# First five pairs of a linear-attention lead-in: order of tail copies, row squares, key exponentials and one quotient

## The chip, the core and the metric

The kernel runs on one core of a Trainium2 chip. The core's engines work side by side and wait for each other through semaphores: TensorE (PE in the rows; PEld is its weight load), VectorE (DVE), ScalarE (ACT), GpSimd (POOL) and SyncE (SP, which here only issues transfers). The metric is the device time of one execution in microseconds (us), lower is better.

## The reference

Random-feature attention over 4 batches x 8 heads, 576 tokens, head size 64, 128 features, followed by two feed-forward layers over all 2304 tokens of width 512 and inner width 2048:

```python
def phi(x):
    proj = np.einsum('bhsd,md->bhsm', x, omega)
    sq = np.sum(x * x, axis=-1, keepdims=True) / 2.0
    h = proj - sq
    h = h - np.max(h, axis=-1, keepdims=True)
    return np.exp(h) / np.sqrt(m)
q_p, k_p = (phi(q_s), phi(k_s))
kv = np.einsum('bhsm,bhsd->bhmd', k_p, v)
z = np.sum(k_p, axis=2)
num = np.einsum('bhsm,bhmd->bhsd', q_p, kv)
den = np.einsum('bhsm,bhm->bhs', q_p, z)[..., None] + 1e-06
...
x = x @ w_in;  g = x * clip(x + 3, 0, 6) / 6;      x = g @ w_out     # first layer
x = x @ w_in2; g = x / (1 + exp(-1.702 * x));      x = g @ w_out2    # second layer
```

## The kernel before

Two heads that lie together are a pair; there are 16. A pair has 576 tokens: four tiles of 128 for each head and a tail of 64, whose two heads share one tile. The feed-forward layers take the tokens in five chunks (four of 512, one of 256) and the inner width in 16 blocks; block `n` has `hidden(n)` (x by w_in) and `output(n)` (g by w_out), each product written as three matmuls of rounded halves (`x_hi`, `x_lo`, `w_hi`, `w_lo`). The four pairs of a batch make up the width of 512, so the first chunk (the first 512 tokens of batch 0) needs pairs 0 to 3 whole. They run in a lead-in with most of pair 4 (`LEAD = 5`), and the rest of pair 4 and pairs 5 to 15 are spread over slots between the blocks.

Each engine runs its own list, written out by hand in one function per engine; what is written is what is issued, and an instruction waits at its place for its semaphores while everything behind it on that engine waits too. For a pair `a` in the lead-in the steps are:

- PE `projection(a, u)` for u = "q", "k" and "tail" (L482, L475): q into banks acc0 and acc1, k into acc2 and acc3, tail into hid0. The next pair's projection waits until the exponentials have read the bank.
- DVE `statistics(a, u)`: row maxima (L864, L861), then two small instructions, `h_max` (L879) and `bias` (L882). Both read two small tiles in SBUF. The half norms they read come from squared rows: ACT squares them (`square_rows`, L671), and for pairs 2 to 4 GpSimd folds them (`fold_rows`, L397 and L399) after both kinds of the pair are squared.
- ACT `exps` (L690, four tiles for each head; L684, the tail), then PE `turn(a, h)` (L504) transposes the query features of head `h`, and ACT `turned_head(a, h)` (L696) copies them back to SBUF.
- PE `key_values(a)` (L510 to L519): transposes the query tail, and for a > 0 the 64 tail tokens of the result of pair a-1 (L513), then sums keys by values. DVE `keep(a)` (L897, L899) copies the sums and the turned tail; `take_tails(a-1)` (L937) copies the pair a-1 tails into `X`.
- PE `quotient(a)` (L533, L536) makes numerators and denominators, DVE `quotient(a)` (L913 to L928) divides, PE `turn_back(a)` (L543) transposes the result, ACT `first_high(a)` (L701) and DVE `first_low(a)` (L942) split it into `x_hi` and `x_lo`.

On PE, `turn(a+1, 0)` waits for `tails_out` and for `take_tails(a-1)`, since it writes over the bank in which the old tails lie. Pair 3 is followed by pieces of `hidden(0, ...)`, which run between `quotient(3)`, the two turns of pair 4, `turn_back(3)` and pair 4's tail projection. `output(0)` writes acc0 to acc3, so it waits bank by bank for pair 4's exponentials: the third and fourth banks hold its key projection. From there on ACT's list per block is `gate(n)` (L753), `high(n)` (L762), attention pieces, and `high_weights` (L729), and DVE's is `gated_block(n)` (L973), attention pieces and `low(n)` (L980).

## Time and profile before

| | us |
|---|---|
| median of three runs | 948.0 |
| lowest and highest of them | 945.12 and 948.49 |
| the profiled execution | 947.79 |
| span between its first and last instruction | 944.9 |
| PE busy within the span | 935.7 |

The span is what the views cover; 2.9 us of the profiled execution lie outside it. Times in a view count from the span's start. In a timeline row the first number is the start, the second the length, and the bracket holds the idle time ahead of it on that engine with what ended it. A matmul's end is modelled, so rows of PE overlap a little and the pitch from one start to the next is the better measure. PEclk is the granted TensorE clock, 1.00 for 2.4 GHz and 0.50 for 1.2 GHz.

### The profile page before, as it was taken

How to read it: one execution, taken by the hardware profiler on the slowest of the kernel's cores; microseconds unless marked ns; L12 is line 12 of the kernel's file. 1: busy time of each engine (PE TensorE's matmuls, PEld its weight loads, DVE VectorE, ACT ScalarE, POOL GpSimd, SP SyncE). 2: the span in 40 equal slices, each digit the busy share in tenths (PEclk: the TensorE clock that was granted, in tenths of full speed). 3: DMA queues.
4: the chain of work that ended last, by engine and by line, in shares of the span. 5: the costliest groups of instructions: out<-in, count | busy, mean ns of one | idle time of the engine just before them, and what ended most of it. 6: DMA issues, size and time to landing. Idle time of an engine off the chain costs nothing.

```text
span 944.9 us, 12973 instructions
## 1 busy us (share of the span) xinstructions
PE 935.7 (99%) x5126; PEld 784.7 (83%) x5126; DVE 398.1 (42%) x734; ACT 381.1 (40%) x871; POOL 170.2 (18%) x182
## 2 busy tenths in 40 slices
PE   8999999999999999999999999999999999999998
PEld 7878788887888778888889988888888888888898
DVE  6856654655546554452224442232223222422332
ACT  7665654554445544442225742232223222322322
POOL 2647455221221210000005830000000000000000
PEclk9999999999999999999999999999999999999999
DMA  8534432212121111010003510001001000100010
GB/s 268 151 89 150 126 106 63 62 39 63 26 63 51 51 26 38 1 45 1 1 0 93 178 43 1 1 1 45 0 1 45 1 1 0 45 1 1 7 39 24
DMA packets 40731, 45.99 MB, mean 49 GB/s; under 512 B 21600, under 2 KB 22240, under 8 KB 40672
## 3 DMA queue, kind: packets, MB, share of 16 engines
q1 hardware_dynamic: 40304, 44.54, 15.5%
q8 instruction: 41, 0.67, 0.3%
q10 hardware_dynamic: 368, 0.62, 0.2%
q14 instruction: 18, 0.15, 0.0%
HBM read 40.44 MB, written 4.72 MB: 48 GB/s over the span
## 4 chain that ended last, share of the span: by engine, by line
PE 97%; DVE 2%; ACT 1%; issue 0%; DVEq 0%
PE acc L616 14%; PE acc L618 14%; PE acc L617 14%; PE hid L593 11%; PE hid L597 10%; PE hid L594 10%; PE att L597 4%; PE att L593 4%; PE att L594 4%; PE att L519 3%; PE att L482 3%; PE att L561 2%; PE att L504 2%; PE acc L482 1%; PE att L475 1%; DVE row_max L864 1%
## 5 line engine op out<-in xcount | busy, mean ns | idle before, releaser
L616 PE MATMUL acc<-g_hi,w_out_hi 128*128 128x512 f32 (+1 forms) x640 | 241.5, 377 | 0.1
L618 PE MATMUL acc<-g_hi,w_out_lo 128*128 128x512 f32 (+1 forms) x640 | 236.2, 369 | 0.0
L617 PE MATMUL acc<-g_lo,w_out_hi 128*128 128x512 f32 (+1 forms) x640 | 235.9, 369 | 0.0
L593 PE MATMUL hid<-x_hi,w_in_hi 128*128 128x512 f32 (+1 forms) x476 | 181.6, 381 | 0.0
L597 PE MATMUL hid<-x_lo,w_in_hi 128*128 128x512 f32 (+1 forms) x476 | 176.0, 370 | 0.4 <-DVE x_lo L965 0.4
L594 PE MATMUL hid<-x_hi,w_in_lo 128*128 128x512 f32 (+1 forms) x476 | 175.4, 369 | 0.0
L980 DVE TENSOR_TENSOR g_lo<-R,g_hi 128x512 fp32r<-128x512 f32 (+1 forms) x160 | 109.0, 681 | 92.4 <-ACT g_hi L762 92.4
L616 PEld LDWEIGHTS acc<-g_hi,w_out_hi 128*128 128x128 f32 x640 | 120.8, 189 | 21.8 <-issue 2.4
L618 PEld LDWEIGHTS acc<-g_hi,w_out_lo 128*128 128x128 f32 x640 | 120.6, 188 | 20.4
L617 PEld LDWEIGHTS acc<-g_lo,w_out_hi 128*128 128x128 f32 x640 | 120.8, 189 | 19.6
L762 ACT ACTIVATE g_hi<-R 128x512 fp32r<-128x512 f32 (+1 forms) x160 | 94.6, 591 | 84.3 <-DVE R L975 52.5
L973 DVE SCALAR_TENSOR_TENSOR R<-R,hid 128x512 f32<-128x512 f32 (+1 forms) x79 | 49.9, 631 | 130.1 <-ACT R L753 130.1
L593 PEld LDWEIGHTS hid<-x_hi,w_in_hi 128*128 128x128 f32 x476 | 89.8, 189 | 16.9 <-issue 0.2
L597 PEld LDWEIGHTS hid<-x_lo,w_in_hi 128*128 128x128 f32 x476 | 89.7, 188 | 16.3 <-DVE x_lo L965 0.8
L594 PEld LDWEIGHTS hid<-x_hi,w_in_lo 128*128 128x128 f32 x476 | 89.8, 189 | 14.4
L753 ACT ACTIVATE R<-hid 128x512 f32<-128x512 f32 (+1 forms) x79 | 43.9, 556 | 106.4 <-PE hid L597 106.3
L975 DVE TENSOR_TENSOR R<-R,hid 128x512 f32<-128x512 f32 (+1 forms) x40 | 25.4, 634 | 113.5 <-ACT R L755 113.5
L975 DVE TENSOR_TENSOR R<-R,att 128x512 f32<-128x512 f32 (+1 forms) x40 | 25.4, 634 | 113.0 <-ACT R L755 113.0
L755 ACT ACTIVATE R<-att 128x512 f32<-128x512 f32 (+1 forms) x40 | 22.2, 555 | 117.0 <-PE att L597 116.4
L755 ACT ACTIVATE R<-hid 128x512 f32<-128x512 f32 (+1 forms) x40 | 22.2, 555 | 116.4 <-PE hid L597 116.4
L948 DVE RECIPROCAL k_phi<-k_phi 128x288 f32<-128x288 f32 x24 | 46.8, 1949 | 38.4 <-ACT k_phi L708 38.4
L594 PE MATMUL att<-x_hi,w_in_lo 128*128 128x512 f32 (+1 forms) x164 | 60.4, 368 | 0.0
(144 smaller groups left out, 1047.9 us busy)
## 6 DMA issues: line engine op xcount, KB each, us to landing
X<-w_in SPq DMA_DIRECT2D x16, 256.0 KB, 2.7
X<-w_out SPq DMA_DIRECT2D x16, 256.0 KB, 2.9
out_t<-X SPq DMA_DIRECT2D x16, 256.0 KB, 2.2
q_cols<-q_t SPq DMA_DIRECT2D x14, 288.0 KB, 2.9
k_cols<-k_t SPq DMA_DIRECT2D x14, 288.0 KB, 3.6
rows<-q_n SPq DMA_DIRECT2D x13, 288.0 KB, 3.6
rows<-k_n SPq DMA_DIRECT2D x13, 288.0 KB, 3.2
v_rows<-v_n SPq DMA_DIRECT2D x14, 256.0 KB, 3.3
```

What stands on the lines that cost most here:

```text
L593: nc.tensor.matmul(bank, w_hi[0][:, at], x_hi[:, k, x0:x0 + t], start=(k == 0), stop=False)
L594: nc.tensor.matmul(bank, w_lo[0][:, at], x_hi[:, k, x0:x0 + t], start=False, stop=False)
L597: last = nc.tensor.matmul(bank, w_hi[0][:, at], x_lo[:, k, x0:x0 + t], start=False, stop=(k == KC - 1))
L616: nc.tensor.matmul(bank, w_hi[1][:, at], g_hi[:, g, 0:t], start=(s == 0), stop=False)
L617: nc.tensor.matmul(bank, w_hi[1][:, at], g_lo[:, g, 0:t], start=False, stop=False)
L618: last = nc.tensor.matmul(bank, w_lo[1][:, at], g_hi[:, g, 0:t], start=False, stop=(s == J - 1))
L755: nc.scalar.activation(R[:, 0:t], h, ACT.Sigmoid, scale=1.702).then_inc(gate_ready, 1)
L762: nc.scalar.activation(g_hi[:, n % G_SLOTS, 0:t], R[:, 0:t], ACT.Copy).then_inc(g_hi_ready, 1)
L948: nc.vector.reciprocal(d, d).then_inc(recip_done, 1)
L973: nc.vector.scalar_tensor_tensor(out=r, in0=r, scalar=6.0, in1=h, op0=ALU.min, op1=ALU.mult).then_inc(gated, 1)
L975: nc.vector.tensor_tensor(r, r, h, ALU.mult).then_inc(gated, 1)
L980: nc.vector.tensor_tensor(g_lo[:, n % G_SLOTS, 0:t], R[:, 0:t], g_hi[:, n % G_SLOTS, 0:t].bitcast(F32), ALU.subtract).then_inc(g_ready, 1)
```

## The change

Five things are moved or recut, all of them in the lead-in; the arithmetic stays.

- DVE copies the old tails (`take_tails`) right behind `keep`, ahead of the key statistics. Pair 4's key statistics move behind `first_low(3)`. For pair 1 the query statistics come ahead of the key maxima.
- ACT squares one kind of rows ahead of `first_high(a)` and the other behind it, both ahead of the next query exponentials. In the start the tail exponentials of pair 0 come ahead of its turned heads.
- ACT takes the key exponentials of a pair in one piece, with the turned heads and the tail behind them; pair 4's come behind `high(0)`. On PE the next key projection moves ahead of `turn(a+1, 1)`.
- PE runs `turn_back(3)` ahead of `turn(4, 1)`, and ACT runs `first_high(3)` ahead of that head's copy.
- DVE's quotient handles the tails first; for pair 3 it is done head by head, with a reciprocal for each.

```diff
--- before.py
+++ after.py
@@ -638,16 +638,16 @@
                 quotient(a)
                 turn(a + 1, 0)
                 projection(a + 2, "q")
+                projection(a + 2, "k")
                 turn(a + 1, 1)
-                projection(a + 2, "k")
                 turn_back(a)
             key_values(LEAD - 2)
             hidden(0, (0,))
             quotient(LEAD - 2)
             turn(LEAD - 1, 0)
             hidden(0, (1,))
+            turn_back(LEAD - 2)
             turn(LEAD - 1, 1)
-            turn_back(LEAD - 2)
             projection(LEAD - 1, "tail")
             hidden(0, (2, 3))
             for n in range(2 * L2):
@@ -785,29 +785,28 @@
             square_rows(0, KK)
             exps_of(0, "q")
             exps_of(0, "k")
+            exps_of(0, "tail")
+            square_rows(1, KQ)
             turned_head(0, 0)
             turned_head(0, 1)
-            exps_of(0, "tail")
-            for a in (1, 2):
-                square_rows(a, KQ)
-                square_rows(a, KK)
+            square_rows(1, KK)
+            square_rows(2, KQ)
+            square_rows(2, KK)
             exps_of(1, "q")
             for a in range(LEAD - 2):
-                exps(a + 1, "k", 0)
+                exps_of(a + 1, "k")
                 turned_head(a + 1, 0)
-                exps(a + 1, "k", 1)
+                exps_of(a + 1, "tail")
                 turned_head(a + 1, 1)
-                exps_of(a + 1, "tail")
-                first_high(a)
-                exps_of(a + 2, "q")
                 if a + 3 < LEAD:
                     square_rows(a + 3, KQ)
+                first_high(a)
+                if a + 3 < LEAD:
                     square_rows(a + 3, KK)
-            exps(LEAD - 1, "k", 0)
+                exps_of(a + 2, "q")
             turned_head(LEAD - 1, 0)
+            first_high(LEAD - 2)
             turned_head(LEAD - 1, 1)
-            first_high(LEAD - 2)
-            exps(LEAD - 1, "k", 1)
             for n in range(2 * L2):
                 former, now = slot_units(2 * n - 1), slot_units(2 * n)
                 for a, what in former:
@@ -833,6 +832,7 @@
                 if n == L2 - 1:
                     nc.scalar.activation(spare[:], ident[:, 0:1], ACT.Sigmoid)
                 if n == 0:
+                    exps_of(LEAD - 1, "k")
                     exps_of(LEAD - 1, "tail")
                 for a, what in now:
                     if what not in ("nd0", "nd1"):
@@ -908,25 +908,34 @@
                 return slice(h * D, (h + 1) * D), slice(at, at + D), slice(at + D, at + D + 1)
 
             def quotient(a):
+
                 tiles = [num_bank(a, h)[:, 0:ST * (D + 1)].rearrange("p (t c) -> p t c", t=ST) for h in range(2)]
-                dve.wait_ge(nd_done, 4 * a + 2)
-                nc.vector.tensor_scalar(dens[:, 0:ST], tiles[0][:, :, D], EPS, None, ALU.add)
-                for h in range(2):
-                    rows_h, _, den = tail_of(h)
-                    nc.vector.tensor_scalar(dens[rows_h, 2 * ST:GROUPS], num_bank(a, 0)[rows_h, den], EPS, None, ALU.add)
-                dve.wait_ge(nd_done, 4 * a + 4)
-                nc.vector.tensor_scalar(dens[:, ST:2 * ST], tiles[1][:, :, D], EPS, None, ALU.add).then_inc(dens_set, 1)
-                dve.wait_ge(dens_set, a + 1)
-                nc.vector.reciprocal(dens[:], dens[:]).then_inc(dens_ready, 1)
-                dve.wait_ge(dens_ready, a + 1)
-                if a > 0:
-                    dve.wait_ge(xs_turned, a)
-                for h in range(2):
-                    rows_h, num, _ = tail_of(h)
-                    nc.vector.tensor_tensor(xs[:, 0:ST, h * D:(h + 1) * D], tiles[h][:, :, 0:D],
-                                            dens[:, h * ST:(h + 1) * ST].unsqueeze(2).to_broadcast([P, ST, D]), ALU.mult)
-                    last = nc.vector.tensor_tensor(xs[rows_h, ST, h * D:(h + 1) * D], num_bank(a, 0)[rows_h, num],
-                                                   dens[rows_h, 2 * ST:GROUPS].to_broadcast([D, D]), ALU.mult)
+                dens_at = (slice(0, ST), slice(ST + 1, GROUPS))
+                tails = slice(ST, ST + 1)
+                parts = ((0,), (1,)) if a == LEAD - 2 else ((0, 1),)
+                for i, heads in enumerate(parts):
+                    for h in heads:
+                        dve.wait_ge(nd_done, 4 * a + 2 * h + 2)
+                        if h == 0:
+                            for side in range(2):
+                                rows_h, _, den = tail_of(side)
+                                nc.vector.tensor_scalar(dens[rows_h, tails], num_bank(a, 0)[rows_h, den], EPS, None, ALU.add)
+                        last = nc.vector.tensor_scalar(dens[:, dens_at[h]], tiles[h][:, :, D], EPS, None, ALU.add)
+                    last.then_inc(dens_set, 1)
+                    dve.wait_ge(dens_set, a + i + 1)
+                    d = dens[:, 0 if 0 in heads else ST + 1:ST + 1 if 1 not in heads else GROUPS]
+                    nc.vector.reciprocal(d, d).then_inc(dens_ready, 1)
+                    dve.wait_ge(dens_ready, a + i + 1)
+                    if a > 0 and i == 0:
+                        dve.wait_ge(xs_turned, a)
+                    for h in heads:
+                        if h == 0:
+                            for side in range(2):
+                                rows_h, num, _ = tail_of(side)
+                                nc.vector.tensor_tensor(xs[rows_h, ST, side * D:(side + 1) * D], num_bank(a, 0)[rows_h, num],
+                                                        dens[rows_h, tails].to_broadcast([D, D]), ALU.mult)
+                        last = nc.vector.tensor_tensor(xs[:, 0:ST, h * D:(h + 1) * D], tiles[h][:, :, 0:D],
+                                                       dens[:, dens_at[h]].unsqueeze(2).to_broadcast([P, ST, D]), ALU.mult)
                 last.then_inc(xs_ready, 1)
 
             def take_tails(a):
@@ -1004,26 +1013,26 @@
                 biases(0, u)
             statistics(0, "tail")
             maxima(1, "q")
-            maxima(1, "k")
             norms(1, KQ)
             biases(1, "q")
+            maxima(1, "k")
             keep(0)
             norms(1, KK)
             biases(1, "k")
             for a in range(LEAD - 2):
                 if a > 0:
                     keep(a)
+                    take_tails(a - 1)
                     statistics(a + 1, "k")
-                    take_tails(a - 1)
                 statistics(a + 1, "tail")
                 quotient(a)
                 statistics(a + 2, "q")
                 first_low(a)
             keep(LEAD - 2)
             take_tails(LEAD - 3)
-            statistics(LEAD - 1, "k")
             quotient(LEAD - 2)
             first_low(LEAD - 2)
+            statistics(LEAD - 1, "k")
             for n in range(2 * L2):
                 before, former, now = (slot_units(2 * n - i) for i in (2, 1, 0))
                 for a, what in former:
```

VectorE, from the copy of pair 1's sums (`keep(1)`) through the key statistics of pair 2 to its tail statistics; L937 and L946 are the copy of the old tails:

```order
 L897 COPY state<-att 128x130
 L899 COPY q_tail_phi_b<-att 128x128
-L864 TENSOR_REDUCE row_max<-acc 128x4 x2
-L879 SCALAR_TENSOR_TENSOR h_max<-row_max,half_norm 128x8
-L882 SCALAR_TENSOR_TENSOR bias<-h_max,half_norm 128x8
-L937 COPY X<-att 64x64 x2
+L946 COPY X<-att 64x64 x2
+L864 TENSOR_REDUCE row_max<-acc 128x4 x2
+L879 SCALAR_TENSOR_TENSOR h_max<-row_max,half_norm 128x8
+L882 SCALAR_TENSOR_TENSOR bias<-h_max,half_norm 128x8
 L861 TENSOR_REDUCE row_max<-hid 128x2
```

The tail copy now stands ahead of three statistics steps instead of behind them; the same happens one pair later.

ScalarE, from the copy of the turned head of pair 1 to the first steps of pair 2 (L671 with X is the squaring of pair 3's rows):

```order
-L690 ACTIVATE k_phi_b<-acc,bias 128x128 x4
-L696 ACTIVATE q_phi_b<-att 128x512
-L690 ACTIVATE k_phi_b<-acc,bias 128x128 x4
+L690 ACTIVATE k_phi_b<-acc,bias 128x128 x8
 L696 ACTIVATE q_phi_b<-att 128x512
 L684 ACTIVATE q_tail_phi_b<-hid,bias 128x128
 L684 ACTIVATE k_phi_b<-hid,bias 128x128
+L696 ACTIVATE q_phi_b<-att 128x512
+L671 ACTIVATE X<-X 128x576
 L701 ACTIVATE x_hi<-att 128x512
+L671 ACTIVATE X<-X 128x576
 L690 ACTIVATE q_phi<-acc,bias 128x128 x8
```

The eight key exponentials stand together, and the two squarings stand on both sides of `x_hi`'s copy instead of behind the query exponentials.

TensorE, in the cycle that turns pair 2 and projects pair 3 (L482 with X):

```order
 L504 MATMUL att<-ident,q_phi 128x128 x4
-L482 MATMUL acc<-omega,X 128x128 x8
+L482 MATMUL acc<-omega,X 128x128 x16
 L504 MATMUL att<-ident,q_phi 128x128 x4
-L482 MATMUL acc<-omega,X 128x128 x8
 L543 MATMUL att<-ident,x_by_token 128x128 x4
 L510 MATMUL att<-ident,q_tail_phi 128x128
```

Both projections now stand between the two turns.

## Rows read from the trace of the kernel before

**Rows 1.** The page's first part: busy time, share of the span, instructions of each engine.

```profile
PE 935.7 (99%) x5126; PEld 784.7 (83%) x5126; DVE 398.1 (42%) x734; ACT 381.1 (40%) x871; POOL 170.2 (18%) x182
```

**Rows 2.** Busy time of the engines by stretch, with granted clock and transfers.

```profile
core 0: us, PE busy (x) PEld busy (x) DVE busy (x) ACT busy (x) POOL busy (x), PEclk, DMA share, GB/s
...
29.60:33.00 3.40, 3.29 (x22) 2.77 (x23) 2.79 (x13) 2.38 (x8) 3.01 (x7) 0.50 0.58 180
...
58.20:944.90 886.70, 883.36 (x4669) 739.29 (x4669) 356.09 (x607) 340.75 (x754) 148.04 (x146) 1.00 0.13 39
```

**Rows 3.** Waits of PE: what for, us in total, times, longest.

```profile
PE att L504 <- ACT q_phi L696: 0.6, 1, 0.6
...
PE att L510 <- ACT k_phi L684: 0.2, 1, 0.2
```

**Rows 4.** Timeline of PE, from the end of quotient(1) to key_values(2).

```profile
27.64 1.00 PE L533 MATMUL att<-state,q_phi_b 128*128 128x65 f32 x8
29.71 1.09 PE L504 MATMUL att<-ident,q_phi 128*128 128x128 f32 x4 [1.07 <-DVE X L937]
30.73 2.08 PE L482 MATMUL acc<-omega,X 64*128 64x128 f32 x16
32.74 0.75 PE L504 MATMUL att<-ident,q_phi 128*128 128x128 f32 x4
...
35.00 0.27 PE L510 MATMUL att<-ident,q_tail_phi 128*128 128x128 f32 x1
```

**Rows 5.** Timeline of PE, the same cycle one pair later.

```profile
39.16 1.00 PE L533 MATMUL att<-state,q_phi 128*128 128x65 f32 x8
41.23 0.63 PE L504 MATMUL att<-ident,q_phi_b 128*128 128x128 f32 x4 [1.07 <-DVE X L937]
41.79 1.16 PE L482 MATMUL acc<-omega,q_cols 64*128 64x128 f32 x16
42.89 0.66 PE L504 MATMUL att<-ident,q_phi_b 128*128 128x128 f32 x4
...
45.26 0.27 PE L510 MATMUL att<-ident,q_tail_phi_b 128*128 128x128 f32 x1
```

**Rows 6.** Timeline of DVE behind key_values(1).

```profile
25.86 0.29 DVE L897 COPY state<-att 128x130 f32<-128x130 f32 x1 [0.86 <-PE att L519]
...
27.65 1.33 DVE L879 SCALAR_TENSOR_TENSOR h_max<-row_max,half_norm 128x8 f32<-128x8 f32 x1
29.01 0.17 DVE L882 SCALAR_TENSOR_TENSOR bias<-h_max,half_norm 128x8 f32<-128x8 f32 x1
29.09 0.47 DVE L937 COPY X<-att 64x64 f32<-64x64 f32 x2
29.59 0.42 DVE L861 TENSOR_REDUCE row_max<-hid 128x2 f32<-128x256 f32 x1
```

**Rows 7.** Timeline of ACT: eight key exponentials, row squares, half the next pair's key exponentials.

```profile
10.82 2.17 ACT L690 ACTIVATE k_phi<-acc,bias 128x128 f32<-128x128 f32 x8
...
26.17 1.31 ACT L671 ACTIVATE X<-X 128x576 f32<-128x576 f32 x2
29.21 1.14 ACT L690 ACTIVATE k_phi<-acc,bias 128x128 f32<-128x128 f32 x4 [1.73 <-DVE bias L882]
```

**Rows 8.** Timeline of POOL, the first step of folding pair 3's rows.

```profile
27.56 1.39 POOL L397 TENSOR_TENSOR X<-X 128x576 f32<-128x576 f32 x1 [2.98 <-ACT X L671]
```

**Rows 9.** Timeline of PE: the second turn of pair 4, and key_values(4).

```profile
52.11 0.63 PE L504 MATMUL att<-ident,q_phi 128*128 128x128 f32 x4 [0.55 <-ACT q_phi L696]
...
61.05 0.27 PE L510 MATMUL att<-ident,q_tail_phi 128*128 128x128 f32 x1
```

**Rows 10.** Timeline of DVE: the low half of pair 3's result, and the gate of block 0.

```profile
53.90 0.69 DVE L942 TENSOR_TENSOR x_lo<-att,x_hi 128x512 fp32r<-128x512 f32 x1 [1.70 <-ACT x_hi L701]
56.02 0.69 DVE L973 SCALAR_TENSOR_TENSOR R<-R,hid 128x512 f32<-128x512 f32 x1 [1.43 <-ACT R L753]
```

**Rows 11.** Timeline of ACT: the high half of block 0, and the gate of block 1.

```profile
56.74 0.63 ACT L762 ACTIVATE g_hi<-R 128x512 fp32r<-128x512 f32 x1 [0.75 <-DVE R L973]
...
59.10 0.59 ACT L753 ACTIVATE R<-att 128x512 f32<-128x512 f32 x1
```

## The prediction

> **What bounds the kernel now.** I read the page's first part, then the busy time by stretch, then PE's own timeline where it is not full. PE is busy 99% of the span [rows 1], and from 58.20 on it is idle 3.3 us in 886.7 [rows 2]. Nothing in that long part is touched but the place of a few ScalarE steps in the first blocks, so the change can be worth only what PE loses in the 58 us ahead of it. That is little: 944.9 - 935.7 = 9.2 us are idle in all, and 3.3 of these lie behind the lead-in, so 5.9 us are idle within it, some 1 us of that before the first instruction. Added to this is one stretch in which PE is busy but slow: from 29.6 to 33.0 the granted clock is 0.50, that is 1.2 GHz, with 1.00 before and behind [rows 2].
>
> The largest waits of PE in the lead-in are the first turn of pair 2 and that of pair 3: each stands 1.07 us until VectorE's copy of the old tails is made (L937) [rows 4, 5]. VectorE makes that copy as the last of four things [rows 6]: the sums at 25.86, the key maxima, h_max and bias until 29.18, and only then the copy at 29.09 to 29.56. These rows are the place at which the change has its effect; the 0.55 us ahead of pair 4's second turn [rows 9] and the 0.2 us ahead of the first key_values [rows 3] are the small ones.
>
> **Part 1: the first pair.** ScalarE's tail exponentials of pair 0 come ahead of its turned heads, so the 0.2 us for which PE's L510 waits go [rows 3]. ScalarE has the same work up to the query exponentials of pair 1, only permuted; VectorE gets the query statistics of pair 1 ready while it would wait. PE's work in the next cycle is the same, and its new wait for all key exponentials of pair 1 is about what the old gap between turn and projection was. Value: -0.25, between 0 and -0.5.
>
> **Part 2: pair 2's turn.** Before, from the end of quotient(1) at 27.64 + 1.00 = 28.64 to key_values(2) at 35.00 are 6.36 us [rows 4]. It holds the wait of 1.07 and the slow clock. The same steps one pair later take 41.23 to 45.26 = 4.03 us at 2.4 GHz, a gap of 0.13 among them [rows 5], so the work itself is 3.9. The price of the slow clock is what the pitches differ by: 29.71 to 30.73 is 1.02 against 0.56, 30.73 to 32.74 is 2.01 against 1.10, and the last turn 0.75 against 0.66 [rows 4, 5]: 0.46 + 0.91 + 0.09 = 1.46 us.
>
> After the change the copy stands behind the sums. From keep's start at 25.86, keep takes 0.4 and the copy 0.5, so it is made at 26.8, while PE is in quotient(1) until 28.64: the wait of 1.07 is gone. What is late next is the key projection of pair 3, which now stands ahead of the second turn and needs all eight key exponentials of pair 2. The chain, in the clock of before: maxima from 26.8 on; from 26.27 they took until 27.65 (the start of h_max, 25.86 + 0.4 is their start), 1.38, so h_max starts at 28.15. h_max and bias take 0.2 each when nothing holds them, the second as in its row [rows 6], so bias is ready at 28.5. ScalarE has been free since the query exponentials and starts within 0.05; eight exponentials take 2.17 [rows 7], until 30.7, and PE follows 0.15 later, at 30.9. PE itself has turned pair 2 and projected its query columns by 28.64 + 0.56 + 1.10 = 30.3, plus a first gap of 0.05. The new wait is therefore 0.5 us. Behind it come the second turn and turn_back, for which the turned head's copy (0.5) and VectorE's quotient are in time.
>
> h_max is not free of risk. Before it took 1.33 us from 27.65 to 28.98 instead of 0.2 [rows 6], and GpSimd's first fold step of pair 3 ran from 27.56 to 28.95 [rows 8]: the two end together. Bias and row maxima next to it kept their length, so I read this as VectorE's instruction with two small inputs in SBUF being held until GpSimd's step ends. The Trainium skill says in "GPSIMD Engine Reference", section 1, Specifications, that GpSimd shares its SBUF interfaces with VectorE and contends with VectorE instructions that have two SBUF inputs. The trace agrees, and adds the size: 1.33 us for one.
>
> This is where the squares matter. The fold starts when ScalarE has squared both kinds. Before, that was behind the query exponentials: 26.17 + 1.31 = 27.5 [rows 7], and the long fold step fell right on h_max. Now the squares lie around x_hi's copy, ahead of the query exponentials that took 2.1 us; the fold starts near 25.3, its step of 1.39 [rows 8] ends near 26.8, before h_max at 28.15, and only the shorter steps behind it can meet h_max and bias. That is 0 to 0.5 us more wait; I take 0.2, so the new wait is 0.7. The query exponentials of pair 2 end 1.3 us later, but PE's turn needs the first half of them only by 28.7 and has it by 26.5.
>
> Cycle after: 3.9 + 0.7 = 4.6 against 6.36: **-1.75**. Of this 1.46 hang on the clock: I count the stretch at 1.2 GHz as gone, since PE had stood still for 1.07 us right ahead of it, and now nothing stands still there. The same idle of 1.07 one pair later did not bring the clock down [rows 5], so idle time alone does not decide, and this is the least safe part of the sum.
>
> **Part 3: pair 3's turn.** Before, from 39.16 + 1.00 = 40.16 to 45.26 are 5.10 us [rows 5], at full clock. After, the same chain gives 4.6: **-0.5**. If h_max and bias meet no fold step it is -0.7, if they meet two it is -0.2.
>
> **Part 4: pair 3's quotient and pair 4.** The wait of 0.55 ahead of pair 4's second turn came from ScalarE, which had the first half of the key exponentials (1.14) ahead of the turned head. Now turn_back(3) stands first and waits for VectorE's quotient. VectorE no longer has pair 4's key statistics (some 1.8 us) ahead of it, but it cannot start before PE has made the numerators; by head it starts 0.8 us earlier and pays one more reciprocal with its handshake (0.25), and its end comes out near 52.0 where it was 52.2. PE stands there 0.6 us, as before: **0**, between -0.3 and +0.3. Behind it, pair 4's key statistics must fit between x_lo and the gate of block 0: x_lo from about 53.4 (53.90 before) for 0.7, then 1.8 us, end near 55.9, against a gate at 56.02 [rows 10]. It fits with 0.1 to spare; what is over comes onto output(0) one to one, 0 to +0.4.
>
> ScalarE now has pair 4's key exponentials behind g_hi: 56.74 + 0.55 + 2.17 = 59.5, and the tail by 60.1. output(0) writes the third accumulator 1.5 us and the fourth 2.2 us behind its start at 58.2, and needs the two halves at 58.4 and 59.5, so it is covered by over 0.8; key_values(4) at 61.05 [rows 9] is covered by 0.9. The gate of block 1 goes from 59.10 [rows 11] to about 61.2, two weight halves with it, and through VectorE's gate to numerators(4) and output(1), which PE reaches at 66 and 68: covered by over 1 us. I cost it at nothing.
>
> **Sum.** -0.25 - 1.75 - 0.5 + 0 = -2.5 us. Against the profiled execution, 947.79 (944.9 of span and 2.9 around it), that is **945.3 us**. The profiled execution is 0.2 under the median of 948.0, so I use it as it is. One of the three runs, 945.12, already lies 2.9 under the median; that spread is as large as the whole effect, and a run without the slow stretch would explain 1.46 of it.
>
> **Rivals.** (a) The slow clock stays or comes elsewhere. For it speaks that the idle ahead of it explains it only once in two cases; the new wait of 0.7 could do the same. Then 1.46 come back: 946.8. (b) The waits only change their name. If the key exponentials end later than I work out, by 0.9 per pair, from x_hi's and VectorE's order together, the two new waits are 1.6 each; with the clock gone this gives 945.3 + 1.8 = 947.1, with it 948.6. (c) Slower: VectorE's h_max and bias are both held by long GpSimd steps. With the fold elsewhere, GpSimd's weight halves follow, of about the length of the long fold step. Two holds of 1.3 make the new wait 0.5 + 2.6 = 3.1 in each of the two cycles instead of 0.7, so 945.3 + 4.8 = 950.1. It decides from a mean wait of 0.7 + 2.5 / 2 = 1.95 per cycle on, above which the kernel is slower than before. Against it: both would need to fall on a long step twice, and the long fold step is moved away. (d) The change does more: no hold at all, and the start's slow phase happens to end earlier, as in the run of 945.12. This gives under 943.5. (e) It does not do what it says: PE's turn waits for something else in place of the copy, such as the query exponentials, which are 1.3 later than before. They are ready 2 us ahead of the turn, so this has hardly a chance of its own and goes with (b).
>
> **How the numbers follow.** The forecast, 944.2 to 946.2, has 0.55; (a) 0.22; (b) with (e) 0.12; (c) 0.06; (d) 0.05. The range of 943.5 to 947.6 holds the forecast, (a) and half of (b), and leaves out (c), most of (d) and the rest of (b), under 2 in 10. A measurement of this kernel can tell about 0.5% from no change, 4.7 us. PE's idle time in the lead-in and the slow stretch together are 7 us, and less than 4 of them are touched, so faster by over 0.5% (under 943.3) has 0.05; slower by over 0.5% (over 952.7) needs (c) and slow stretches besides, 0.02; the rest is within, 0.93.
>
> **What would show it.** Right: no wait of L504 for the tail copy, in its place one of the key projection (L482) for the key exponentials of 0.5 to 1.0 us, twice; the fold of pair 3 about 2 us earlier and h_max near 0.2 to 0.5 us; PEclk 1.00 from 26 to 45; key_values(3) at about 42.8 instead of 45.26; the gate of block 0 about 2.5 us earlier than 56.02, straight behind pair 4's key statistics. Wrong: a stretch at 0.50, an h_max over 1 us with the fold or a weight half beside it, PE waiting at key_values(4) or in output(0), or a PE idle time after the first block other than 3.3 us.

## The result

The changed kernel takes 943.8 us (median of 12 runs, 943.67 to 944.36), the kernel before 945.89 (12 runs, 944.77 to 948.91). The ratio is 0.997, with an interval from 0.9959 to 0.9981: faster by 0.3%, which the interval sets apart from no change, but less than the 0.5% that I had called the least that can be told. The time is 1.5 us under the forecast of 945.3: it lies in the outer range of 943.5 to 947.6, but below the 944.2 to 946.2 in which I expected it. Repeated beside three experiments the changed kernel took 944.43 (12 runs, 943.72 to 944.89; ratio 0.9978, 0.997 to 0.9987).

A second thing changed, and it is needed to read the numbers. The runs of the kernel before lie in two groups: five of these 12 between 948.0 and 948.9, seven between 944.8 and 946.0, nothing between. In the last comparison it was 7 of 23 above 947.8. The changed kernel has one group, 24 runs of 24 below 944.9 (counting the repetition). The execution that I predicted from, 947.79, is of the upper group.

The busy time by stretch of the changed kernel (columns as in [rows 2]) shows that the stretch at 1.2 GHz is gone. The profiled execution took 943.76, its span is 941.3.

```profile
26.00:29.60 3.60, 3.31 (x36) 2.95 (x35) 3.21 (x14) 2.49 (x11) 3.13 (x8) 1.00 1.02 283
29.60:33.00 3.40, 2.90 (x33) 2.81 (x33) 2.85 (x7) 2.48 (x8) 2.70 (x3) 1.00 0.58 189
...
55.00:941.30 886.30, 882.90 (x4669) 738.85 (x4667) 354.97 (x607) 342.30 (x760) 147.28 (x146) 1.00 0.13 39
```

PE's idle time behind the lead-in is 3.4 us, where it was 3.3 [rows 2]: all of the difference lies ahead of it. Its waits, changed kernel (what for, us in total, times, longest):

```profile
PE acc L482 <- ACT k_phi L690: 1.3, 2, 0.8
...
PE acc L482 <- ACT k_phi_b L690: 1.0, 2, 0.8
PE att L543 <- DVE x_by_token L937: 0.5, 1, 0.5
```

The waits for the tail copy are gone. In their place stands one of 0.8 in each cycle for the key exponentials, at the key projection (the rest of these two rows, 0.5 and 0.2, is ahead of the two cycles), and 0.5 for the divided tokens where there were 0.55 for the turned head [rows 9]. PE's timeline of the cycle of [rows 4], and the two key_values behind it:

```profile
26.77 1.00 PE L533 MATMUL att<-state,q_phi_b 128*128 128x65 f32 x8
27.61 0.61 PE L504 MATMUL att<-ident,q_phi 128*128 128x128 f32 x4
28.15 1.16 PE L482 MATMUL acc<-omega,X 64*128 64x128 f32 x16
30.10 1.16 PE L482 MATMUL acc<-omega,X 64*128 64x128 f32 x16 [0.79 <-ACT k_phi L690]
31.20 0.65 PE L504 MATMUL att<-ident,q_phi 128*128 128x128 f32 x4
31.69 0.60 PE L543 MATMUL att<-ident,x_by_token 128*128 128x128 f32 x4
32.12 0.27 PE L510 MATMUL att<-ident,q_tail_phi 128*128 128x128 f32 x1
...
41.64 0.27 PE L510 MATMUL att<-ident,q_tail_phi_b 128*128 128x128 f32 x1
```

The turn follows the quotient without a gap. Behind the key_values of pair 3, at 41.64, PE reaches output(0) after 12.93 us (12.95 before), and from there both kernels take 886.7 us.

### The profile page after: what moved, and what is told of

Read it like the earlier page. It is cut to its first block, busy times and chain, and to the rows that moved or that the text cites. A ratio compares the mean times of both kernels' runs of the same rounds, so it can differ in the third digit from the quotient of the medians.

```text
span 941.3 us, 12974 instructions
## 1 busy us (share of the span) xinstructions
PE 932.8 (99%) x5126; PEld 782.8 (83%) x5126; DVE 394.3 (42%) x735; ACT 380.5 (40%) x871; POOL 169.9 (18%) x182
## 4 chain that ended last, share of the span: by engine, by line
PE 96%; DVE 2%; ACT 2%; issue 0%; DVEq 0%
PE acc L616 14%; PE acc L617 14%; PE acc L618 14%; PE hid L593 11%; PE hid L597 10%; PE hid L594 10%; PE att L593 4%; PE att L594 4%; PE att L597 4%; PE att L519 3%; PE att L482 3%; PE att L561 2%; PE att L504 1%; PE att L475 1%; DVE row_max L864 1%; PE acc L482 0%
## 5 line engine op out<-in xcount | busy, mean ns | idle before, releaser
L616 PE MATMUL acc<-g_hi,w_out_hi 128*128 128x512 f32 (+1 forms) x640 | 241.5, 377 | 0.1
L616 PEld LDWEIGHTS acc<-g_hi,w_out_hi 128*128 128x128 f32 x640 | 120.7, 189 | 21.8 <-issue 2.4
L593 PE MATMUL att<-x_hi,w_in_hi 128*128 128x512 f32 (+1 forms) x164 | 60.4, 368 | 0.0
```

The lines of the kernel that those rows point to most:

```text
L593: nc.tensor.matmul(bank, w_hi[0][:, at], x_hi[:, k, x0:x0 + t], start=(k == 0), stop=False)
L616: nc.tensor.matmul(bank, w_hi[1][:, at], g_hi[:, g, 0:t], start=(s == 0), stop=False)
```

## A ruler for the experiments

The first key_values starts at a time that varies by up to 1 us from one execution of a kernel order to the next, and by 2.2 us in the profiled execution of tails_alone; the first transfers and the speed of the first projection (16 matmuls in 1.29 us in b_again, in 1.99 in tails_alone) differ already. So each profiled execution is also read from key_values(0) to the start of output(0), with the cycles between key_values(1), (2) and (3), all as starts of L510 and of the first L616 in PE's timeline:

| kernel | median, us | cycle 1 to 2 | cycle 2 to 3 | key_values(0) to output(0) |
|---|---|---|---|---|
| before, upper group ([rows 3 to 5, 9]) | 948.2 | 11.52 | 10.26 | 43.68 |
| before, lower group (b_again) | 945.7 | 10.26 | 9.17 | 41.62 |
| changed | 943.8 | 9.51 | 9.52 | 40.80 |
| tails_alone | 946.50 | 10.14 | 10.14 | 42.18 |
| squares_old | 945.40 | 10.13 | 10.14 | 42.03 |
| split_exps | 944.18 | 9.47 | 9.47 | 40.81 |
| fourth_old | 944.36 | 9.50 | 9.52 | 40.78 |
| tails_old | 942.95 | 8.93 | 8.95 | 39.66 |
| maxima_tails_old | 942.94 | 8.45 | 9.12 | 39.35 |
| maxima_early | 942.43 | 8.45 | 8.45 | 38.67 |
| maxima_all | 942.12 | 8.45 | 8.45 | 38.24 |

(For the two groups of before, the times are the medians of the 28 and 58 runs of each group that were taken beside the experiments. The other medians come from different chips, so differences of a few tenths are read from the last column.) One unit of the last column is one unit of time: what lies behind output(0) is 886.7 to 886.8 us in all.

Two things stand outside this ruler. From the first turn to key_values(0) the kernel before takes 4.7 us (9.84 to 14.53, and 9.86 to 14.56 in b_again), the changed kernel 4.4 (9.38 to 13.77): another 0.3 of gain, which is part 1's. And the time outside the span is 2.35 to 2.63 us in all 24 runs of the changed kernel, but 2.73 to 3.03 in 77 of 86 runs of the kernel before, and in 6 of 8 runs of fourth_old below. No run shows where these 0.4 us come from.

## Experiments on the kernel before

**b_again**: the kernel before, once more and without an edit, to catch an execution of the other group.

> The kernel before, unchanged. Its twelve runs so far lie in two groups, five between 948.0 and 948.9 and seven between 944.8 and 946.0; the changed kernel's twelve lie between 943.7 and 944.4. Theory: the upper group is the executions with a stretch at 1.2 GHz behind the 1.07 us wait of the first turn (the profiled one of before had it from 29.6 to 33.0). Then the two groups appear again, and a profiled execution of about 945.4 shows no such stretch, while one of about 948.4 does. Rival: the groups come from elsewhere (start, transfers); then both kinds of profile look alike in PEclk.

12 runs, median 945.83 (945.39 to 948.48), two of them above 947.4. The mean granted clock of every run, kept with its time, ties the groups to the clock: of the 86 runs of the kernel before that were taken here and beside the other experiments, the 28 with a mean of 0.998 are exactly those from 947.58 up, and the 58 with 0.999 or 1.000 lie at 946.58 or below. The profiled one took 945.83. PE in the cycle of [rows 5], which there had 1.07 of waiting for the tail copy:

```profile
37.93 1.00 PE L533 MATMUL att<-state,q_phi 128*128 128x65 f32 x8
38.84 0.63 PE L504 MATMUL att<-ident,q_phi_b 128*128 128x128 f32 x4
39.40 1.16 PE L482 MATMUL acc<-omega,q_cols 64*128 64x128 f32 x16
```

DVE and POOL beside it, with the query bias that comes earlier on DVE:

```profile
34.15 1.15 DVE L882 SCALAR_TENSOR_TENSOR bias<-h_max,half_norm 128x8 f32<-128x8 f32 x1
...
37.93 0.17 DVE L879 SCALAR_TENSOR_TENSOR h_max<-row_max,half_norm 128x8 f32<-128x8 f32 x1
38.14 0.17 DVE L882 SCALAR_TENSOR_TENSOR bias<-h_max,half_norm 128x8 f32<-128x8 f32 x1
38.22 0.47 DVE L937 COPY X<-att 64x64 f32<-64x64 f32 x2
```

```profile
34.00 1.27 POOL L417 TENSOR_TENSOR w_out_lo<-X,w_out_hi 128x512 fp32r<-128x512 f32 x1
38.73 3.59 POOL L397 TENSOR_TENSOR rows<-rows 128x576 f32<-128x576 f32 x5 [3.45 <-ACT rows L671]
```

The clock is 1.00 throughout this execution. The first cycle has its wait of 1.07 as before and is 1.26 shorter than in the upper group; that is the price of the slow stretch (I had 1.46). But the second cycle is 1.09 shorter as well, and nothing in it is slow: h_max takes 0.17 because the fold begins 0.8 behind it, and so the copy is made in time. Counted from key_values(2), h_max starts at 4.17 in the execution of [rows 5] and at 4.16 here, but the fold at 4.08 there (39.08) and at 4.96 here. The fold follows ScalarE's query exponentials, and here these waited for a query bias that one of GpSimd's weight halves held until 35.30. GpSimd keeps its pace while PE is slow (the weight half at 32.06 in the one and at 32.10 in the other take 1.26 us each): in the execution of [rows 5] the one that holds the bias here started 1.04 us ahead of key_values(2) (33.96), here 0.23 behind it, and so it met another instruction. So a stretch at 1.2 GHz in the first cycle costs its own 1.26 and then 1.09 for a wait that it brings about in the next, of which 0.29 comes back behind key_values(3) (12.95 us to output(0) against 13.24 here): 2.06 in all. The same 1.07 stood in both cycles of my rows, and I took it for a property of the kernel.

**fill_wait** and **fill_short**: the kernel before with matmuls on PE in the wait ahead of the turn.

```diff
                 quotient(a)
+                if a > 0:                 # fill_short: if a == 1
+                    pe.wait_ge(exp_done, banks_to(a + 1, "q", 1))
+                    warm(8, acc[0])       # fill_short: warm(4, acc[0])
                 turn(a + 1, 0)
```

> The kernel before with eight idle-filling matmuls of 128 columns (about 0.13 us each) on PE ahead of the first turn of pair 2 and of pair 3, where it waits 1.07 us; they write a bank that is free then, and no order is changed. Theory (idle PE ahead of the turn brings the clock down): the waits cost the same, but the upper group is gone, all runs 945.0 to 946.2, PEclk 1.00 from 26 to 45. Rival (the stretch has another cause): two groups as in the kernel before, some runs over 948.

12 runs, median 947.63 (946.96 to 950.07), ratio 1.002 (1.001 to 1.0029). Neither expectation fits. Eight fillers take 1.84 us (28.10 to 29.94), not 1.07, and the second cycle had no wait to hide them in: both cycles are 10.83 or 10.84. The times alone don't tell whether a group is missing; the granted clock does in part: eleven of the twelve have a mean of 1.000 and one, 950.07, has 0.998, where 28 of 86 would have been about four. The filler has to fit.

> The kernel before with four filling matmuls of 128 columns on PE ahead of pair 2's first turn only, where it waits 1.07 us in both kinds of execution (29.71 and 29.74). Eight of them took 1.84 us from first start to the turn, so four take about 0.92 and fit into the wait. Theory (the idle there brings the clock to 1.2 GHz in part of the executions, and the upper group is these): no run, or one of twelve, above 947.4, where the kernel before has some 4 in 10, and a median of 945.4 to 946.0. Rival (the upper group has another cause): 4 or 5 of twelve above 947.4.

12 runs, median 946.16, 945.45 to 947.28, none above 947.4, where the kernel before had 7 of 23 beside it on the same chip. PE's timeline:

```profile
28.17 1.11 PE L491 MATMUL acc<-state 128*128 128x128 f32 x8
29.40 0.63 PE L504 MATMUL att<-ident,q_phi 128*128 128x128 f32 x4
```

The turn starts when it did, and its stretch from key_values(0) to output(0) is 41.62, as in b_again. What is taken away is only the idle time, and with it the upper group. All twelve have a granted clock of 1.000. With 28 of 86 runs in the upper group, twelve without one would come up by chance about once in a hundred times (an estimate from these two counts). That is the evidence that PE's idle time ahead of this turn brings on the slow stretch, in a part of the executions. What tells these from the others was not found; the upper end of this kernel's runs, 947.28, lies higher than the lower group's.

**tails_alone**: of the whole change only the tail copy is moved.

```diff
                     keep(a)
+                    take_tails(a - 1)
                     statistics(a + 1, "k")
-                    take_tails(a - 1)
```

> The kernel before with one part of the change alone: the old tails are copied right behind the sums. Theory of the prediction's sum (the copy is what PE waits for): the two waits of 1.07 go, about 2 us less than the lower group of before, 943.4. Rival (the chain of key statistics and key exponentials stands right behind it and takes the wait over; the copy alone also delays that chain by 0.5, while the fold's long step still lies on h_max): at most 0.3 us per cycle is gained, 944.9 to 945.5, with PE waiting for exponentials at the key projection instead. Either way the upper group should be gone if the idle ahead of the turn makes the clock drop, since the idle moves behind a projection.

12 runs, median 946.5 (945.87 to 948.56), ratio 0.9996 (0.9987 to 1.0006). The rival was right that the copy's move gains nothing, but its 944.9 to 945.5 was too low. Both cycles are 10.14, their sum 20.28 against 19.43 in b_again; 0.29 of these 0.85 comes back behind key_values(3), and to output(0) 0.56 is lost. Eleven of the twelve runs have a granted clock of 1.000. The twelfth, 948.56, is the profiled one: its slow stretch lies not here but at the start, behind 1.99 us in which PE waited for the first key columns (6.57 to 8.56), and the ruler does not hold it.

```profile
9.00:14.00 5.00, 5.00 (x40) 4.38 (x38) 2.95 (x8) 4.36 (x17) 0.00 (x0) 0.66 1.02 288
```

PE's waits:

```profile
PE att L504 <- ACT q_phi L696: 1.4, 2, 0.8
...
PE att L504 <- ACT q_phi_b L696: 0.8, 1, 0.8
...
PE acc L482 <- ACT k_phi L690: 0.4, 1, 0.4
PE acc L482 <- ACT k_phi_b L690: 0.4, 1, 0.4
```

VectorE's h_max in the first cycle:

```profile
30.38 0.84 DVE L879 SCALAR_TENSOR_TENSOR h_max<-row_max,half_norm 128x8 f32<-128x8 f32 x1
```

In the first cycle the copy ahead of the statistics costs nothing: h_max starts 0.5 later than in b_again but is held to the end of the same fold step, and counted from key_values(1) (25.71 here, 23.51 there) the key exponentials start at 5.75 (31.46) against 5.74 (29.25). PE's wait only changes its name, and the cycle is 0.12 shorter. In the second cycle the half microsecond moves h_max from ahead of the fold (b_again) to under it (0.83 in place of 0.17), and the cycle is 0.97 longer.

## Experiments on the changed kernel

**changed_again**: the changed kernel without an edit; its result is given above.

> The changed kernel, unchanged, beside the three others on one chip. 943.8 with one group of runs, 943.6 to 944.6; both theories of the other runs take it as their base.

**tails_old**: the tail copy back behind the key statistics, all else as changed.

```diff
                     keep(a)
-                    take_tails(a - 1)
                     statistics(a + 1, "k")
+                    take_tails(a - 1)
```

> The changed kernel with the tail copy put back behind the key statistics, all else as changed. Theory of the sum (the copy bound the turn): PE waits about 1 us for the copy again at both turns, 945.8. Rival (with the squares moved, h_max is short, so the copy would be made only 0.3 us after PE arrives, and the key exponentials start 0.5 us earlier than in the changed kernel): PE waits 0.35 at the turn and hardly at the key projection, 943.8 - 0.9 = 942.9 to 943.4.

5 runs, median 942.95 (942.77 to 943.54), ratio to the kernel before 0.996 (0.9948 to 0.9973). The rival by its number, though PE's wait at the turn is 0.1 where it had 0.35. VectorE:

```profile
25.45 1.28 DVE L864 TENSOR_REDUCE row_max<-acc 128x4 f32<-128x512 f32 x2
26.84 0.19 DVE L879 SCALAR_TENSOR_TENSOR h_max<-row_max,half_norm 128x8 f32<-128x8 f32 x1
27.06 0.17 DVE L882 SCALAR_TENSOR_TENSOR bias<-h_max,half_norm 128x8 f32<-128x8 f32 x1
27.14 0.47 DVE L946 COPY X<-att 64x64 f32<-64x64 f32 x2
```

The copy is made at 27.61 and PE's turn starts at 27.75, 0.1 later than the changed kernel's relative to key_values(1). From the start of the first projection to the second turn PE then takes 28.31 to 30.68 = 2.37, where the changed kernel takes 28.15 to 31.20 = 3.05. Each cycle is 0.57 to 0.58 shorter. So the part of the change that I had put in its centre costs 1.1 us here, where h_max is short: as tails_alone shows, it costs nothing while h_max is held to the same step's end.

**squares_old**: both squarings back behind the query exponentials.

```diff
-                if a + 3 < LEAD:
-                    square_rows(a + 3, KQ)
                 first_high(a)
+                exps_of(a + 2, "q")
                 if a + 3 < LEAD:
+                    square_rows(a + 3, KQ)
                     square_rows(a + 3, KK)
-                exps_of(a + 2, "q")
```

> The changed kernel with both squarings back behind the next query exponentials. Theory (a fold step of 1.39 us that falls on h_max holds it): the fold starts near 26.8 and h_max at 27.3 ends with its first step near 28.2; the two waits for exponentials grow from 0.79 to about 1.5, 943.8 + 1.4 = 945.2, x_hi's copy being earlier without use. Rival (the hold is chance or harmless): 943.8 within 0.3.

11 runs, median 945.4 (945.08 to 946.12), ratio 0.9984 (0.9975 to 0.9993). By the number of the theory. DVE and POOL:

```profile
28.30 0.88 DVE L878 SCALAR_TENSOR_TENSOR h_max<-row_max,half_norm 128x8 f32<-128x8 f32 x1
29.21 0.17 DVE L881 SCALAR_TENSOR_TENSOR bias<-h_max,half_norm 128x8 f32<-128x8 f32 x1
```

```profile
27.75 1.40 POOL L397 TENSOR_TENSOR X<-X 128x576 f32<-128x576 f32 x1 [2.62 <-ACT X L671]
```

h_max ends at 29.18, the fold's step at 29.15, and PE waits 1.41 for the exponentials in each cycle. The place of the squares is worth 1.23 us from key_values(0) to output(0), about as much as the changed kernel gains over the lower group.

**split_exps**: key exponentials in two halves around the turned head, PE's second turn ahead of the key projection.

```diff
-                exps_of(a + 1, "k")
+                exps(a + 1, "k", 0)
                 turned_head(a + 1, 0)
-                exps_of(a + 1, "tail")
+                exps(a + 1, "k", 1)
                 turned_head(a + 1, 1)
+                exps_of(a + 1, "tail")
...
-                projection(a + 2, "k")
                 turn(a + 1, 1)
+                projection(a + 2, "k")
```

> The changed kernel with the key exponentials of pairs 1 to 3 again in two halves around the turned head, and PE's second turn again ahead of the key projection. Theory: the end of the chain is the same, since the copy of the turned head (0.5 us) only changes place with a turn on PE (0.5 us): 943.6 to 944.1. Rival (one piece matters): 0.5 us per cycle slower, 944.8.

9 runs, median 944.18 (943.87 to 945.13), ratio 0.9979 (0.9969 to 0.9988). No difference beyond that of the runs: PE waits 0.16 and 0.40 in place of 0.79, and the cycles are 9.47.

**fourth_old**: quotient(3) in one piece and everything of pair 4 in its old order, on PE, ScalarE and VectorE.

```diff
             hidden(0, (1,))
-            turn_back(LEAD - 2)
             turn(LEAD - 1, 1)
+            turn_back(LEAD - 2)
...
+            exps(LEAD - 1, "k", 0)
             turned_head(LEAD - 1, 0)
-            first_high(LEAD - 2)
             turned_head(LEAD - 1, 1)
+            first_high(LEAD - 2)
+            exps(LEAD - 1, "k", 1)
...
                 if n == 0:
-                    exps_of(LEAD - 1, "k")
...
-                parts = ((0,), (1,)) if a == LEAD - 2 else ((0, 1),)
+                parts = ((0, 1),)
...
+            statistics(LEAD - 1, "k")
             quotient(LEAD - 2)
             first_low(LEAD - 2)
-            statistics(LEAD - 1, "k")
```

> The changed kernel with everything of pairs 3 and 4 behind keep(3) as before: quotient in one piece, key statistics of pair 4 ahead of it, second turn ahead of turn_back, key exponentials of pair 4 ahead of the gate of block 0. Theory (one wait of 0.5 us for another): 943.8 within 0.2. Rival (the part gains on its own): 944.2 to 944.5.

8 runs, median 944.36 (943.95 to 945.09), ratio 0.9977 (0.9966 to 0.9987). No difference that can be measured: 40.78 to output(0) against 40.80, with the old wait of 0.6 for the turned head in place of 0.5 for the tokens.

## A faster version

The new wait ends a chain of maxima, h_max, bias and eight exponentials, while VectorE stands idle for 1.07 us ahead of first_low. **maxima_early** puts the maxima there, for pairs 2 and 3:

```diff
                     take_tails(a - 1)
-                    statistics(a + 1, "k")
+                    biases(a + 1, "k")
...
                 statistics(a + 2, "q")
+                if a < LEAD - 3:
+                    maxima(a + 2, "k")
                 first_low(a)
```

> The changed kernel with one more move: VectorE takes the row maxima of the next pair's keys ahead of first_low, in an idle of 1 us there, for pairs 2 and 3; h_max and bias stay behind the tail copy. Theory (the new waits of 0.79 at the key projection are the end of the chain maxima, h_max, bias, eight exponentials): the chain is 1.3 us shorter, the two waits go, 943.8 - 1.5 = 942.3, perhaps 0.1 to 0.3 of it lost since x_lo comes a little later. Rival (the wait is set by ScalarE's query exponentials that end at 26.5, or h_max then falls on the fold's long step at 24.7 to 26.1): half of it or less, 943.0 to 943.8.

6 runs, median 942.43 (941.48 to 942.66), ratio to the kernel before 0.9954 (0.9941 to 0.9967). Both cycles are 8.45, and PE waits in neither:

```profile
27.91 0.61 PE L504 MATMUL att<-ident,q_phi 128*128 128x128 f32 x4
28.44 2.06 PE L482 MATMUL acc<-omega,X 64*128 64x128 f32 x32
30.43 0.65 PE L504 MATMUL att<-ident,q_phi 128*128 128x128 f32 x4
```

**maxima_all** does the same for pair 4, in VectorE's idle ahead of first_low(3), and lets PE's second turn go ahead of turn_back(3) again, since it is ready first.

```diff
             hidden(0, (1,))
-            turn_back(LEAD - 2)
             turn(LEAD - 1, 1)
+            turn_back(LEAD - 2)
...
-            first_high(LEAD - 2)
             turned_head(LEAD - 1, 1)
+            first_high(LEAD - 2)
...
             quotient(LEAD - 2)
+            maxima(LEAD - 1, "k")
             first_low(LEAD - 2)
-            statistics(LEAD - 1, "k")
+            biases(LEAD - 1, "k")
```

> The kernel maxima_early with two more moves around pair 4: the second turn again ahead of turn_back(3) on PE, with its copy ahead of first_high(3) on ScalarE, and the row maxima of pair 4's keys ahead of first_low(3) on VectorE, in its idle of 1.4 us. Theory (PE stands 0.5 us for the divided tokens while the turn could run, and the gate of block 0 must not be delayed by the key statistics): 0.4 us under maxima_early, 942.0. Rival (the end of the chain through x_hi, x_lo is what counts): the same as maxima_early, 942.4.

5 runs, median 942.12 (941.32 to 942.37), ratio 0.9951 (0.9936 to 0.9966), against 944.43 for the changed kernel on the same chip. From key_values(0) to output(0) it is 38.24, 0.43 under maxima_early, as expected; the medians of five and six runs differ by 0.3, which they can't carry alone. VectorE around the moved maxima:

```profile
47.14 1.28 DVE L864 TENSOR_REDUCE row_max<-acc 128x4 f32<-128x512 f32 x2
48.63 0.69 DVE L951 TENSOR_TENSOR x_lo<-att,x_hi 128x512 fp32r<-128x512 f32 x1 [0.21 <-ACT x_hi L701]
```

**maxima_tails_old** is maxima_early with the tail copy behind h_max and bias.

```diff
-                    take_tails(a - 1)
                     biases(a + 1, "k")
+                    take_tails(a - 1)
```

> The kernel maxima_early with the tail copy behind h_max and bias instead of ahead of them. Theory (which of the two stands first matters only while one of them is what PE waits for; with the maxima early PE waits for neither): the same as maxima_early, 942.4 within 0.3. Rival (the tail copy belongs behind the key statistics in any case, as the gain of tails_old over the changed kernel suggests): 0.3 or more lower.

5 runs, median 942.94 (942.36 to 943.43), ratio 0.9961 (0.9946 to 0.9976). Both expectations miss. The first cycle is 8.45, the second 9.12, with a wait that no other kernel has:

```profile
35.42 1.08 PE L533 MATMUL att<-state,q_phi 128*128 128x65 f32 x8 [0.72 <-DVE q_tail_phi L899]
```

VectorE and POOL ahead of it:

```profile
31.96 1.17 DVE L882 SCALAR_TENSOR_TENSOR bias<-h_max,half_norm 128x8 f32<-128x8 f32 x1
33.05 1.28 DVE L864 TENSOR_REDUCE row_max<-acc 128x4 f32<-128x512 f32 x2
34.25 0.68 DVE L951 TENSOR_TENSOR x_lo<-att,x_hi 128x512 fp32r<-128x512 f32 x1
34.85 0.28 DVE L897 COPY state<-att 128x130 f32<-128x130 f32 x1
```

```profile
31.83 1.27 POOL L417 TENSOR_TENSOR w_out_lo<-X,w_out_hi 128x512 fp32r<-128x512 f32 x1
```

The query bias of pair 3 is held until a weight half ends (33.13 and 33.10). The maxima, x_lo and the copy of the sums stand behind it, and now that the maxima fill VectorE's idle time there is none left to take it up. In maxima_early the same bias started before that weight half, at 31.40, and took 0.17. The traces show what put it there: counted from key_values(1), the fold's first step starts at 2.07 in both kernels, but h_max at 3.28 in maxima_early, behind the tail copy, and at 2.78 here. It is held to the end of that step in both, for 0.22 there and 0.71 here, and VectorE reaches the tail statistics of pair 2 at 3.74 there and at 4.11 here. So the tail copy ahead of h_max is of use in this kernel: it is done in time that h_max would spend held. At pair 3's query bias 0.14 us of that delay is left (0.18 behind key_values(2) against 0.04), just enough to come behind the start of the weight half and into the next hold, which shows that the faster versions have little room there.

## Why the prediction came out as it did

Against the profiled execution that it was made from, point by point (starts in PE's timeline):

| step | forecast | measured |
|---|---|---|
| first pair, up to key_values(1) | -0.25 | -0.87, of it 0.46 because the first turn starts earlier (9.84 and 9.38), ahead of everything that the change touches |
| pair 2's cycle | -1.75 | 11.52 to 9.51: -2.01 |
| pair 3's cycle | -0.5 | 10.26 to 9.52: -0.74 |
| pair 3's quotient, pair 4, to output(0) | 0 | -0.02 |
| from there to the end of the span | 0 | 0.0 |
| outside the span | 0 | 2.9 to 2.5: -0.4 |
| sum | -2.5 | -4.0 |

- **What held.** The steps on PE went as written: no wait at the turn, a new one of 0.8 (forecast 0.7) at the key projection, the fold of pair 3 at 24.68 instead of 27.56 and h_max at 0.26 instead of 1.33, the full clock, no wait at key_values(4), nothing behind the lead-in, and part 4 at zero.
- **The miss of 1.5 us.** By the table it is made of three things: the two cycles (0.5), the first pair (0.6, of which 0.46 is that execution's start and the rest part 1, which the order made 0.41 instead of 0.25), and the time outside the span (0.4), which the sum had at nothing without a reason and whose cause stays open.
- **Sizes of the cycles.** Each came out 0.25 shorter than forecast. The step that failed is "from the end of quotient(1) at 27.64 + 1.00 = 28.64": a matmul's modelled end. A turn that does not wait starts 0.84 behind the start of the last quotient matmuls (26.77 and 27.61), not 1.00. And in the new order the cycle's work from the turn's start is 32.12 - 27.61 = 4.51 less the gap of 0.85 ahead of the second projection, 3.66, where I had taken 3.9 from the old order. Together 0.4 less, against a new wait that is 0.15 longer than the 0.7 of the sum.
- **The base.** The step that failed is "The profiled execution is 0.2 under the median of 948.0, so I use it as it is". Both are of the upper group, which has 3 or 4 runs in 10. Against the lower group's median in the same comparison (945.4) the gain is 1.6 us, and in the later one (945.6 against 944.43) 1.2. The traces agree: 41.62 to 40.80 is 0.8 between key_values(0) and output(0), 0.3 more lies ahead of key_values(0), and 0.4 outside the span. The span of b_again is 1.6 longer than the changed kernel's, but 0.48 of that is again the start (9.86 and 9.38). I had seen the run of 945.12 and written that a run without the slow stretch explains 1.46; it explains 1.26 and, through the hold that the stretch causes in the next cycle, 0.8 more. That the sum of -2.5 lies near the 2.1 between the two medians is luck: 1.46 of it is for a slow stretch that two thirds of the runs don't have.
- **The cause.** The step that failed is "These rows are the place at which the change has its effect". The copy was late in [rows 6] because h_max was held 1.16 us ahead of it. Take the hold away, and the copy behind the statistics is 0.1 late (tails_old). Put it ahead, and it delays the chain that PE waits for next. I had this hold in the text as a risk to the new order, and not as the reason of the old wait. What gains is the place of the squares: 1.23 with the copy ahead (squares_old), 1.96 from b_again to tails_old, which have the copy behind (the second step holds the small parts of the change too). The tail copy's move costs 1.14, and its merit is that no idle time stands ahead of the turn any more, a merit that tails_old has as well.
- **The rivals.** None came. (b) had a wait that changes its name, which is what happened and what the sum has too, but with too large a size.

## What to carry to other kernels

A wait for the last of several things in a row on one engine says nothing about the order among them: look first for the instruction in that row that took far longer than its like, and for what ran beside it. Work that is put ahead of a held instruction can be free, and the same work ahead of one that is not held is paid in full. Before one engine's chain is put in another order, work out which chain stands next behind the wait, since what is moved ahead delays it by its whole length. And where the runs of a kernel fall into groups, find out to which one the profile belongs before its time is made the base of a sum.

## What the runs showed of the hardware

VectorE's instructions with two small inputs in SBUF (0.17 us) were held to the end of the GpSimd step beside them in every alignment seen: 28.98 and 28.95 in [rows 6, 8], 29.18 and 29.15 in squares_old, 33.13 and 33.10 in maxima_tails_old, for steps of 1.27 to 1.40 us. Over all 14 traces, h_max or bias starts 214 times under a GpSimd step (a fold, a rounding or a weight half) with at least 0.2 us of it left, and every one ends 0.02 to 0.03 us behind the step. Those that start ahead of a step, or with none beside them, take 0.13 to 0.17. The row maxima (0.68 us for each of the two) and the copies out of PSUM beside the same steps kept their length. What I had not expected is that one such hold decides over the next: an early shift of 1.2 us, from a clock stretch, made a hold one pair later appear or vanish.

The granted clock fell to 1.2 GHz from 29.6 on behind 1.07 us without a matmul, in some executions and not in others of the same kernel (b_again has the same idle time at 1.00), and with four filling matmuls in that idle time no run of twelve was in the upper group. In the profiled execution of tails_alone it was at 1.2 GHz from 10 to 13, behind 1.99 us without a matmul and then some 1.2 us of work. What decides in which executions it falls is not shown.
